# GpSimd's low parts of the second chunk's gate input move ahead of the low parts of a late-weight piece

## The chip, the cores and the metric

The program runs on one core of one Trainium2 chip. The metric is the device time of one execution in microseconds (us), lower is better. A core has a matrix engine (TensorE, PE in the rows), a vector engine (VectorE, DVE), an activation engine (ScalarE, ACT), GpSimd (POOL) and a queue engine (SyncE, SP) that issues transfers between memory and the on-chip SBUF. Each works through its own list of instructions in order, and they wait for one another by semaphores. TensorE writes into PSUM, a second on-chip memory.

## The reference

Three layers follow one another. The first is an attention of 2 × 8 heads over 768 tokens with head size 64, in which a query sees only keys of its own hash bucket. Its output, as 2 × 768 tokens of 512 features, is `x` of the second layer:

```
for k in range(K): gate_pre += conv_w[k] * xp[:, k:k + S, :]   # causal, K = 5 taps
gate = 1.0 / (1.0 + np.exp(-gate_pre))
val = x @ w_val
return gate * val @ w_out
```

The third layer takes that as `x`, with `x_prev` its tokens moved by one:

```
xk = mu_k * x + (1.0 - mu_k) * x_prev
xr = mu_r * x + (1.0 - mu_r) * x_prev
k = np.maximum(xk @ w_k, 0.0)          # 512 -> 1024
v = k * k @ w_v                        # 1024 -> 512
r = 1.0 / (1.0 + np.exp(-(xr @ w_r)))
return r * v
```

## The kernel before

Every fp32 matrix product is made of three products of rounded halves: an operand `a` is split into `a_hi`, a rounded copy, and `a_lo = a - a_hi`, and hi·hi, hi·lo and lo·hi are summed in PSUM. ScalarE makes most high parts, GpSimd most low parts, so each operand of TensorE passes ScalarE and then GpSimd.

The first 245 us or so are the attention, 16 heads in 8 pairs. The rest works on six chunks of 256 tokens, c = 0 to 5. Per chunk TensorE runs, with its matmuls of 128 × 256: **val** (`x @ w_val`, 48 of them), **k** (96), **r** (48), **out** (`y @ w_out`, 48, of the chunk ahead) and **v** (96). Its order is val(0), the last attention product, out(0), then for each c: val(c+1), k(c), r(c), out(c+1), v(c). All three single-pass stages and k share line 702, v is line 710.

Around the change, where attention hands over to the chunks, the work stands so:

- **GpSimd**: the gates of chunks 0 and 1 (`gates`, L416), then the low parts of `y` of chunk 0 (`y_low`, L421, four tiles), with the low parts of pieces 0 and 1 of `w_v` (`w2_low`, L411, one instruction of 128 × 1024 each) put between and behind them, then `x_low(1)` (L358, 128 × 1024), the low part of the second chunk's input, then `s_out(0)` (L432): eight instructions of 128 × 256, `xk_lo` and `xr_lo` by turns for four feature tiles.
- **VectorE**: it normalises the last head (L881), waits for z, and in its own `s_out(0)` runs three instructions for each tile: `tmp_b = z - z_prev` (L958), `tmp_a = mu_k * tmp_b + z_prev` (L960), `tmp_b = mu_r * tmp_b + z_prev` (L963). Later it takes the low parts of pieces 2 and 3 of `w_v` itself (L1006).
- **ScalarE**: `x_hi(1)` (L506), the high part of piece 1 (`w_hi<-w_raw`, L599), then z out of PSUM (L572), `xk_hi` and `xr_hi` (L566), and the high parts of pieces 2 and 3.
- **TensorE**: val(1) waits for `xlo_done`, which `x_low(1)` raises; k(0) waits for `mixlo_done` to stand at 7, so for the last `xk_lo`.
- **SyncE**: `w_v` comes in four pieces of 512 KB through two buffers (L301). Piece n ≥ 2 waits for `w2lo_done[0]` to stand at n - 1: piece 2 for `w2_low(0)`, piece 3 for `w2_low(1)`.

Of the kernel before, what the change touches and what calls it, by code (L numbers as in the profile page):

```python
# [88 lines left out]
def build(nc, qT, kT, v, proj, w1, w2, conv, mu_k, mu_r, codes, rows, out):  # L89
    ctx = ExitStack()  # L90
    with ctx:
# [80 lines left out]
        def w2_piece(halves, n):  # L172
            return halves[n // 2][:, n % 2 * W2_PIECE:(n % 2 + 1) * W2_PIECE]
# [51 lines left out]
        def x_tokens(c, first=HALO):  # L225
            b, n = divmod(c, CPB)
            return x[:, b * DT:(b + 1) * DT, first + n * GQ:first + (n + 1) * GQ]
# [82 lines left out]
        def _(pool):  # L310
# [45 lines left out]
            def x_low(c):  # L356
                pool.wait_ge(xhi_done, c + 1)
                pool.tensor_tensor(x_lo[:, :, :], x_tokens(c), x_hi[:, :, :], ALU.subtract).then_inc(xlo_done, 1)  # L358
# [50 lines left out]
            def w2_low(n):  # L409
                pool.wait_ge(w2hi_done, n + 1)  # L410
                pool.tensor_tensor(w2_piece(w2_lo, n), w2_raw[:, n, :], w2_piece(w2_hi, n), ALU.subtract)\  # L411
                    .then_inc(w2lo_done[0], 1)
# [6 lines left out]
            def y_low(c, m):  # L419
                pool.wait_ge(yhi_done, c * DT + m + 1)  # L420
                pool.tensor_tensor(y_lo[:, m, :], tmp_a[:, m % 2, :], y_hi[:, m, :], ALU.subtract)\  # L421
                    .then_inc(ylo_done, 1)
# [5 lines left out]
            def s_out(c):  # L428
                for m in range(DT):
                    for n, (hi, lo, tmp) in enumerate(((xk_hi, xk_lo, tmp_a), (xr_hi, xr_lo, tmp_b))):  # L430
                        pool.wait_ge(mixhi_done, (c * DT + m) * 2 + n + 1)
                        pool.tensor_tensor(lo[:, m, :], tmp[:, m % 2, :], hi[:, m, :], ALU.subtract)\  # L432
                            .then_inc(mixlo_done, 1)
# [16 lines left out]
            w2_low(0)  # L450
            y_low(0, 2)
            y_low(0, 3)
            w2_low(1)
            pool.wait_ge(mm["val"], DT)
            x_low(1)
            s_out(0)
            for c in range(CHUNKS):
                if c + 1 < CHUNKS:
# [628 lines left out]
```

## Time and profile before

| | |
|---|---|
| time, median of 3 runs | 485.42 us (482.16 to 485.42) |
| the profiled execution's own time | 484.38 us |
| its span in the trace | 482.2 us |
| TensorE busy | 468.8 us, 97% |
| VectorE busy | 352.0 us, 73% |
| ScalarE busy | 274.5 us, 57% |
| GpSimd busy | 252.2 us, 52% |
| chain that ended last | PE 72%, DVE 15%, issue 7%, the rest below 3% each |

The span is from the first to the last instruction in the trace; the execution's own time has 2.2 us more around it. "Busy" counts matmuls that overlap in the pipeline. The granted clock is TensorE's, as a share of full speed (2.4 GHz); 0.50 is its lower level (1.2 GHz). The chain that ended last is followed back from the last instruction, at each step to what released it.

### The profile page before, as it was taken

How to read it: one execution, taken by the hardware profiler on the slowest of the kernel's cores; microseconds unless marked ns; L12 is line 12 of the kernel's file. 1: busy time of each engine (PE TensorE's matmuls, PEld its weight loads, DVE VectorE, ACT ScalarE, POOL GpSimd, SP SyncE). 2: the span in 40 equal slices, each digit the busy share in tenths (PEclk: the TensorE clock that was granted, in tenths of full speed). 3: DMA queues.
4: the chain of work that ended last, by engine and by line, in shares of the span. 5: the costliest groups of instructions: out<-in, count | busy, mean ns of one | idle time of the engine just before them, and what ended most of it. 6: DMA issues, size and time to landing. Idle time of an engine off the chain costs nothing.

```text
span 482.2 us, 9463 instructions
## 1 busy us (share of the span) xinstructions
PE 468.8 (97%) x3493; PEld 398.3 (83%) x3493; DVE 352.0 (73%) x624; ACT 274.5 (57%) x581; POOL 252.2 (52%) x242
## 2 busy tenths in 40 slices
PE   7899999999999999999998999999999999999997
PEld 5766667676676767667778999999999999999997
DVE  5888898989889899888657877876668579326211
ACT  4977877787787887876535541442443353344230
POOL 5786447284553637360377573575455457346140
PEclk9999999999999999999998999999999999999999
DMA  6202414013041311211140001001000000100101
GB/s 231 67 19 71 154 34 153 21 46 131 26 154 35 133 38 29 77 35 34 60 149 2 0 2 45 1 1 44 1 1 27 19 1 2 45 1 1 45 0 46
DMA packets 13885, 23.89 MB, mean 50 GB/s; under 512 B 2960, under 2 KB 10256, under 8 KB 13840
## 3 DMA queue, kind: packets, MB, share of 16 engines
q1 hardware_dynamic: 13552, 23.14, 14.7%
q8 instruction: 28, 0.46, 0.4%
q10 hardware_dynamic: 288, 0.15, 0.1%
q14 instruction: 17, 0.14, 0.1%
HBM read 20.08 MB, written 3.19 MB: 48 GB/s over the span
## 4 chain that ended last, share of the span: by engine, by line
PE 72%; DVE 15%; issue 7%; POOL 2%; ACT 2%; DMA 1%; DVEq 0%; SPq 0%; ACTq 0%; POOLq 0%
PE ps L702 28%; PE ps L710 11%; PE ps L690 11%; PE ps L664 10%; PE ps L675 9%; DVE pt L851 2%; DVE gate L891 2%; DVE negmax L844 2%; DVE k L836 2%; DVE tmp_a L960 2%; DVE tmp_b L958 1%; DVE tmp_b L983 1%; PE ps L647 1%; DVE x L881 1%; PE ps L638 1%
## 5 line engine op out<-in xcount | busy, mean ns | idle before, releaser
L844 DVE TENSOR_REDUCE negmax<-ps 128x1 f32<-128x768 f32 x96 | 91.6, 956 | 16.0 <-PE ps L664 15.3
L484 ACT ACTIVATE probs<-ps,negmax 128x768 f32<-128x768 f32 x96 | 86.6, 902 | 15.7 <-DVE negmax L844 15.4
L664 PE MATMUL ps<-k,q 128*128 128x384 f32 x384 | 92.5, 362 | 3.1 <-ACT probs L484 2.8
L675 PE MATMUL ps<-ident,probs 128*128 128x128 f32 x576 | 83.7, 275 | 2.5 <-DVE pt L851 1.3
L664 PEld LDWEIGHTS ps<-k,q 128*128 128x128 f32 x384 | 62.6, 189 | 24.7 <-ACT probs L484 20.4
L675 PEld LDWEIGHTS ps<-ident,probs 128*128 128x128 f32 x576 | 67.7, 140 | 11.9 <-DVE pt L851 7.5
L690 PE MATMUL ps<-pt,vals 128*64 128x384 f32 x384 | 68.8, 494 | 0.0
L438 POOL TENSOR_TENSOR h_lo<-tmp_b,h_hi 128x256 fp32r<-128x256 f32 x48 | 39.3, 824 | 45.2 <-ACT h_hi L579 45.2
L492 ACT ACTIVATE pt<-ps 128x384 f32<-128x384 f32 x96 | 46.9, 488 | 23.3 <-PE ps L675 21.3
L702 PE MATMUL ps<-xk_hi,w_hi 128*128 128x256 f32 x192 | 54.6, 285 | 1.9 <-POOL xk_lo L432 1.9
L702 PE MATMUL ps<-xk_lo,w_hi 128*128 128x256 f32 x192 | 54.6, 284 | 0.0
L702 PE MATMUL ps<-xk_hi,w_lo 128*128 128x256 f32 x192 | 54.5, 284 | 0.0
L851 DVE COPY pt<-ps 128x384 f32<-128x384 f32 x96 | 52.1, 543 | 2.5 <-PE ps L675 2.5
L710 PE MATMUL ps<-h_hi,w_hi 128*128 128x256 f32 x192 | 53.4, 278 | 0.0
L710 PE MATMUL ps<-h_lo,w_hi 128*128 128x256 f32 x192 | 53.3, 278 | 0.0
L710 PE MATMUL ps<-h_hi,w_lo 128*128 128x256 f32 x192 | 53.3, 278 | 0.0
L891 DVE SCALAR_TENSOR_TENSOR gate<-x,conv_sb,gate 128x256 f32<-128x256 f32 x96 | 50.2, 523 | 1.5
L690 PEld LDWEIGHTS ps<-pt,vals 128*64 128x64 f32 x384 | 24.8, 136 | 31.2 <-issue 31.1
L337 POOL TENSOR_TENSOR q<-raw_q,q 64x768 fp32r<-64x768 f32 x16 | 29.2, 1826 | 39.9 <-DVE gate L891 28.6
L983 DVE TENSOR_TENSOR tmp_b<-tmp_a 128x256 f32<-128x256 f32 x48 | 32.2, 671 | 22.5 <-ACT tmp_a L586 21.8
L702 PEld LDWEIGHTS ps<-xk_hi,w_hi 128*128 128x128 f32 x192 | 37.0, 193 | 2.1 <-POOL xk_lo L432 2.1
L702 PEld LDWEIGHTS ps<-xk_lo,w_hi 128*128 128x128 f32 x192 | 37.2, 194 | 0.0
(84 smaller groups left out, 1090.2 us busy)
## 6 DMA issues: line engine op xcount, KB each, us to landing
w_raw<-w SPq DMA_DIRECT2D x8, 640.0 KB, 5.3
raw_q<-qT SPq DMA_DIRECT2D x8, 384.0 KB, 4.0
raw_k<-kT SPq DMA_DIRECT2D x8, 384.0 KB, 3.7
vals<-v SPq DMA_DIRECT2D x16, 192.0 KB, 2.5
r_sb<-rows SPq DMA_DIRECT2D x32, 96.0 KB, 2.7
out<-w_raw SPq DMA_DIRECT2D x24, 128.0 KB, 1.7
w_raw<-w SPq DMA_DIRECT2D x4, 512.0 KB, 4.2
rows<-r_rows SPq DMA_DIRECT2D x64, 0.8 KB
```

Source lines behind the costliest of these rows:

```text
L438: pool.tensor_tensor(h_lo[:, m, :], tmp_b[:, m % 2, :], h_hi[:, m, :], ALU.subtract)\
L484: act.activation(probs[par][:, :], score[par], ACT.Exp, bias=negmax[:, t:t + 1], accum_out=sums[:, t, 0:1]).then_inc(exp_done, 1)
L492: act.activation(pt[head % 2][:, 0:3, tt * P:(tt + 1) * P], tbank3[0], ACT.Copy).then_inc(up_done[0], 1)
L664: last = pe.matmul(ps[:, 2 * par + half, 0:HALF], qq[h][:, q], kk[h][:, half * HALF:(half + 1) * HALF], start=first, stop=not first)
L675: last = pe.transpose(tbank[u][:, k * P:(k + 1) * P], probs[g % 2][:, kt * P:(kt + 1) * P], ident[:, :])
L690: last = pe.matmul(ps[DH * n:DH * (n + 1), 6, 0:HALF], vals[h][:, kt, :], pt[h][:, kt, n * HALF:(n + 1) * HALF], start=kt == 0, stop=kt == ...
L702: last = pe.matmul(ps[:, bank, 0:GQ], wt[:, w], act_in[:, kt, :], start=(kt == 0 and n == 0), stop=(kt == kts - 1 and n == 2))
L710: last = pe.matmul(ps[:, m, 0:GQ], wt[half][:, first:first + P], act_in[:, kt, :], start=(kt == 0 and n == 0), stop=(kt == FT - 1 and n == 2))
L844: dve.tensor_reduce(negmax[:, t:t + 1], score[g % 2], AX.XY, ALU.max, negate=True).then_inc(max_done, 1)
L851: dve.tensor_copy(pt[head % 2][:, 3:6, tt * P:(tt + 1) * P], tbank3[1]).then_inc(up_done[1], 1)
L891: ins = dve.scalar_tensor_tensor(to, src, conv_sb[:, m, k:k + 1], to, ALU.mult, ALU.add)
L983: dve.tensor_tensor(tmp_b[:, m % 2, :], tmp_a[:, m % 2, :], tmp_a[:, m % 2, :], ALU.mult)\
```

## The change

In GpSimd's list the wait for val(0) and `x_low(1)` stand ahead of `w2_low(1)` and no longer behind it. No instruction is added or removed, and the lists of the other engines are as before.

```diff
@@ -450,9 +450,9 @@
             w2_low(0)
             y_low(0, 2)
             y_low(0, 3)
-            w2_low(1)
             pool.wait_ge(mm["val"], DT)
             x_low(1)
+            w2_low(1)
             s_out(0)
```

GpSimd's list at that place, before; `w_lo<-w_raw,w_hi` is `w2_low`, its first row piece 0 and its second piece 1, `x_lo` is `x_low(1)`:

```order
 L421 TENSOR_TENSOR y_lo<-tmp_a,y_hi 128x256 x2
 L411 TENSOR_TENSOR w_lo<-w_raw,w_hi 128x1024
 L421 TENSOR_TENSOR y_lo<-tmp_a,y_hi 128x256 x2
 L411 TENSOR_TENSOR w_lo<-w_raw,w_hi 128x1024
 L358 TENSOR_TENSOR x_lo<-x,x_hi 128x1024
 L432 TENSOR_TENSOR xk_lo<-tmp_a,xk_hi 128x256
 L432 TENSOR_TENSOR xr_lo<-tmp_b,xr_hi 128x256
```

And the difference that the change makes there, the only one on any engine:

```order
 L411 TENSOR_TENSOR w_lo<-w_raw,w_hi 128x1024
 L421 TENSOR_TENSOR y_lo<-tmp_a,y_hi 128x256 x2
+L358 TENSOR_TENSOR x_lo<-x,x_hi 128x1024
 L411 TENSOR_TENSOR w_lo<-w_raw,w_hi 128x1024
-L358 TENSOR_TENSOR x_lo<-x,x_hi 128x1024
 L432 TENSOR_TENSOR xk_lo<-tmp_a,xk_hi 128x256
 L432 TENSOR_TENSOR xr_lo<-tmp_b,xr_hi 128x256
```

`x_lo` has moved past one instruction and past its wait for piece 1's high part; piece 1's low part now stands behind the wait for val(0) and for `x_hi(1)`.

## Rows read from the trace of the kernel before

**Rows 1.** Waits of TensorE, whole span: who for whom, us in total, times, longest.
```profile
PE ps L664 <- ACT probs L484: 2.8, 3, 1.7
PE ps L702 <- POOL xk_lo L432: 1.9, 1, 1.9
...
PE ps L702 <- ACT recept L595: 0.2, 1, 0.2
```

**Rows 2.** The chain that ended last, 245 to 280: start us, us, what.
```profile
249.25 2.50 DVE tmp_a L960
...
259.35 19.62 PE ps L702 x156
```

**Rows 3.** Timeline of GpSimd: start us, us, what, idle before it and its releaser.
```profile
242.51 1.41 POOL L421 TENSOR_TENSOR y_lo<-tmp_a,y_hi 128x256 fp32r<-128x256 f32 x2
246.52 2.40 POOL L411 TENSOR_TENSOR w_lo<-w_raw,w_hi 128x1024 fp32r<-128x1024 f32 x1 [2.60 <-ACT w_hi L599]
248.88 2.58 POOL L358 TENSOR_TENSOR x_lo<-x,x_hi 128x1024 fp32r<-128x1024 f32 x1
...
258.39 0.91 POOL L432 TENSOR_TENSOR xk_lo<-tmp_a,xk_hi 128x256 fp32r<-128x256 f32 x1
```

**Rows 4.** Timeline of VectorE, chunk 0 and the same step of chunk 1.
```profile
245.38 1.14 DVE L881 TENSOR_TENSOR x<-ps,r_sb 64x384 f32<-64x384 f32 x2 [3.61 <-PE ps L690]
...
247.48 1.73 DVE L958 TENSOR_TENSOR tmp_b<-z 128x256 f32<-128x256 f32 x1 [0.83 <-ACT z L572]
249.25 2.49 DVE L960 SCALAR_TENSOR_TENSOR tmp_a<-tmp_b,mu_sb,z 128x256 f32<-128x256 f32 x1
251.77 0.49 DVE L963 SCALAR_TENSOR_TENSOR tmp_b<-tmp_b,mu_sb,z 128x256 f32<-128x256 f32 x1
...
279.57 2.23 DVE L958 TENSOR_TENSOR tmp_b<-z 128x256 f32<-128x256 f32 x1 [3.43 <-ACT z L572]
281.83 0.48 DVE L960 SCALAR_TENSOR_TENSOR tmp_a<-tmp_b,mu_sb,z 128x256 f32<-128x256 f32 x1
```

**Rows 5.** Timeline of GpSimd in chunk 1's step.
```profile
279.12 2.39 POOL L358 TENSOR_TENSOR x_lo<-x,x_hi 128x1024 fp32r<-128x1024 f32 x1
```

**Rows 6.** Timeline of TensorE at val(1) and k(0).
```profile
250.90 0.28 PE L702 MATMUL ps<-y_hi,w_lo 128*128 128x256 f32 x1
251.51 0.38 PE L702 MATMUL ps<-x_hi,w_hi 128*128 128x256 f32 x1 [0.33 <-POOL x_lo L358]
...
257.15 0.28 PE L702 MATMUL ps<-x_hi,w_lo 128*128 128x256 f32 x1
259.35 0.39 PE L702 MATMUL ps<-xk_hi,w_hi 128*128 128x256 f32 x1 [1.92 <-POOL xk_lo L432]
...
260.28 0.40 PE L702 MATMUL ps<-xk_lo,w_hi 128*128 128x256 f32 x1
...
263.68 0.31 PE L702 MATMUL ps<-xk_hi,w_lo 128*128 128x256 f32 x1
```

**Rows 7.** By stretch: busy us of each engine, then TensorE's granted clock, DMA.
```profile
11.00:13.00 2.00, 0.32 (x3) 0.08 (x1) 2.00 (x3) 1.12 (x3) 2.00 (x2) 1.00 0.00 0
...
260.00:265.00 5.00, 5.00 (x32) 5.00 (x32) 3.21 (x6) 2.51 (x6) 3.19 (x4) 0.66 0.01 3
```

**Rows 8.** Timeline of ScalarE.
```profile
242.13 1.04 ACT L506 ACTIVATE x_hi<-x 128x1024 fp32r<-128x1024 f32 x1
245.39 1.06 ACT L599 ACTIVATE w_hi<-w_raw 128x1024 fp32r<-128x1024 f32 x1 [2.21 <-DMA w_raw<-w]
...
259.07 1.99 ACT L599 ACTIVATE w_hi<-w_raw 128x1024 fp32r<-128x1024 f32 x2
...
277.92 1.05 ACT L506 ACTIVATE x_hi<-x 128x1024 fp32r<-128x1024 f32 x1
```

**Rows 9.** VectorE's normalising line: durations in ns, min/median/max, all 32.
```profile
L881 DVE TENSOR_TENSOR x<-ps,r_sb x32: 549/556/561, 39.9 to 246.0; 64x384 f32<-64x384 f32 x32
```

**Rows 10.** The page's transfer issues: KB each, median us to landing.
```profile
w_raw<-w SPq DMA_DIRECT2D x4, 512.0 KB, 4.2
```

## The prediction

> **What bounds the kernel now.** The table of busy times shows TensorE at 97%, so I first read where it still waits. Its waits over the whole span [rows 1] name, from the hand-over of the attention to the chunks on, only three worth a look: 1.9 us for `xk_lo` at the start of k(0), 0.33 us for `x_lo` at the start of val(1) [rows 6], and 0.2 us for `recept` at out(2). Everything behind k(0) is matmul after matmul, so what k(0) wins in start time comes out at the end, unless a slower loop on the other engines takes it back.
>
> Next, the chain of waits: before k(0) it does not run through TensorE but through VectorE's `tmp_a` (L960) of the first tile, 2.50 us, and after it through 156 matmuls, 19.62 us [rows 2]. The same instruction takes 0.48 us one chunk later [rows 4]. The reader is to see why by laying the timelines of the two engines beside each other [rows 3, 4]. `tmp_b` starts at 247.48, while GpSimd runs `w_lo` (246.52 to 248.92), and ends at 249.21, 0.29 us behind it. `tmp_a` starts at 249.25, while GpSimd runs `x_lo` (248.88 to 251.46), and ends at 251.74, 0.28 us behind it. In chunk 1 there is one long GpSimd instruction only, `x_lo` from 279.12 to 281.51 [rows 5]; there `tmp_b` takes 2.23 us and ends at 281.80, 0.29 us behind it, and `tmp_a` is free. So a VectorE instruction with two SBUF inputs is held until GpSimd's current one is over, and in chunk 0 that happens twice, since two long ones stand back to back. VectorE, ScalarE and GpSimd then run the four tiles to the last `xk_lo`, at 258.39 + 0.91 = 259.30, and k(0) starts at 259.35 [rows 3, 6].
>
> Last, the granted clock by stretches: it is 0.66 of full between 260 and 265 [rows 7], and single matmuls show it: 16 steps from 260.28 to 263.68, 0.2125 us each, against (257.15 - 251.51)/47 = 0.120 in val(1), 0.118 without its first, longer step [rows 6]. That is the lower level, right behind the gap of 1.92 us.
>
> **The change, term by term.** One GpSimd instruction of 2.4 us passes another; nothing is added.
>
> *`x_lo` in its new place.* It needs the y parts before it (over at 243.92, rows 3), `x_hi(1)` (over at 243.17, rows 8) and val(0), which was done before `x_hi(1)` began, since ScalarE waits for it there. GpSimd was idle for 2.60 us just here, waiting for piece 1's high part [rows 3], so `x_lo` runs at 243.9 to 246.3, at 2.39 us [rows 5]; nothing else uses that time. Stretched by 0.2 us, as the 2.58 in its old place, it ends at 246.5.
>
> *`w2_low(1)`.* Its high part is ready at 245.39 + 1.06 = 246.45 [rows 8] and it started at 246.52; between `x_lo`'s end at 246.3 or 246.5 and that there is 0 to 0.2 us left, so it stays where it was, within 0.1. So does the transfer of piece 3 that it releases at 248.92: at 4.2 us to landing [rows 10] it is in by 253.2, while ScalarE takes it up, with all earlier by 2.0, at 257.1 [rows 8]. Cover 3.9 us, cost nothing.
>
> *val(1).* `x_lo` is five us ahead of need. val(1) began 0.61 us behind the last matmul of out(0), where 0.12 is the step: 0.49 earlier. Alone this is worth nothing, because k(0) waits for `xk_lo` and its gap would only grow.
>
> *The first tile on VectorE.* `tmp_b` still sits behind `w_lo` and ends at 249.21; `tmp_a` has no long GpSimd instruction beside it: 0.48 for 2.49, so it ends 2.01 us earlier. Behind it, the cascade keeps its steps if z comes in time: the third z needs the third tile of out(0), whose last matmul is at about 250.90 - 12 × 0.118 = 249.5, and is wanted at 250.6; the fourth has more room. So the last `xk_lo` ends at 257.3 and k(0) starts at 257.35: **-2.0 us**. The bounds: nothing, if the hold isn't what makes `tmp_a` long, and -2.0; I take the latter, as chunk 1 shows this very pair of instructions with one hold.
>
> *The gap and the clock.* TensorE's last val(1) matmul starts at 256.66, 0.49 earlier, and ends at 256.94. The gap is 0.4 us instead of 1.92. I expect no fall of the clock behind it: 16 matmuls win 0.0945 each, -1.5. Against that stands the spacing of the matmuls that follow: 132 steps from 263.68 to the last of the 156 took 0.1137 each [rows 2, 6], closer than the 0.118 of val(1), and I can't tell whether that comes back without the fall. At 0.118 throughout, the 156 take 156 × 0.118 + 0.3 = 18.7 for 19.62: **-0.9 us**; at 0.1137 it is 18.0: -1.6. I take the first, from the stretch nearest in kind and time. If the clock falls all the same, the term is 0.
>
> *The loop behind it.* VectorE's square steps of k(0) and its low parts move by 2.0 with the start, the rest by what TensorE gives: it was idle 3.43 us before the first z of out(1) [rows 4], and 2.4 of it stay, so z sets its pace there, and that follows TensorE through ScalarE's `x_hi(2)` (1.05 us, rows 8). Both then are 2.9 to 3.0 earlier, and the 0.2 us at out(2) stays what it was, give or take. Behind that nothing is changed.
>
> Sum: -2.0 - 0.9 = **-2.9 us**, so 481.5 for the profiled execution (span 482.2 to 479.3, own time 484.38). The median of the runs is 1.04 above that execution: 485.42 - 2.9 = **482.5 us**.
>
> **Rivals.**
>
> 1. *The clock falls all the same*, somewhere in k(0). For: one fall after one gap is a thin base, and in the first 15 us a gap of 1.7 us (the longest for `probs`, rows 1) left the clock at 1.00 [rows 7], so the gap of 1.92 alone may not be the cause. Against: no fall is to be seen in any stretch where TensorE is not held. Only the -2.0 is left: 483.4. The Trainium skill (TensorE: Matmul & The Clock Gate, "Why this matters for your kernels") warns only of idle gaps clearly longer than the one here, so by it this gap didn't bring the clock down and closing it needn't keep it up; no run yet shows which.
>
> 2. *The fall is worth more.* The runs lie 3.3 us apart. If the lowest is one without a fall in k(0), and after the change all are like it, they come to 482.16 less the 2.0 of the hold: 480.2, with the closer spacing 480.0. For: a spread of this size fits one or two falls of 1.5. Against: nothing in one profile says which runs had them.
>
> 3. *The hold isn't the cause, or moves on*: `tmp_a` stays at 2.5. Then val(1) is early, k(0) starts as before, gap 2.4: 485.4. Against it stand three instructions that end 0.28 to 0.29 us behind GpSimd's.
>
> 4. *Slower: the normalising step is held instead.* VectorE's L881 starts its two halves at 245.38, now beside `x_lo`. If its first half waits for `x_lo` and its second for `w_lo`, it ends at 248.92 + 0.56 = 249.5. TensorE wants it for the third tile of out(0) at 250.90 - 23 × 0.118 = 248.2. From there on it decides: idle 1.3 us, and if the clock falls for that gap too, 1.5 more; val(1)'s last matmul is at 256.66 + 2.8 = 259.5, k(0) starts at 259.6 for 259.35, and with the fall in k(0) as before the end is 485.7. Against: its 32 instructions take 549 to 561 ns, held by none of GpSimd's [rows 9]; one of their two inputs is in PSUM. The Trainium skill (GPSIMD Engine Reference, "Key points") names contention for VectorE instructions with two SBUF inputs, and that would leave this one alone; the rows agree.
>
> **Chances and range.** Forecast 0.57; rival 1, 0.18; rival 2, 0.15; rival 3, 0.07; rival 4, 0.03. The change lies between 0 and -5.2 us. A measurement of this kernel tells about 1% (4.9 us) from no change. Only rival 2 gets past it, and not always, since its 480.0 to 480.2 is just past 480.6: faster 0.13. Slower by 1% has no case: 0.02. Same 0.85. The range takes in the forecast with both spacings (481.8 to 482.5), rival 1 and rival 2, and stops short of rival 3, but with the runs' own scatter: 480.0 to 484.8.
>
> **What would show it.** `x_lo` at 243.9 and `w_lo` still at 246.5 on GpSimd; `tmp_a` at 0.5 us; k(0) from 257.3 behind a gap of 0.4; clock 1.00 between 258 and 263; out(1)'s first z about 3 us earlier; the wait at out(2) still small. Wrong would be: `tmp_a` still 2.5 us (rival 3), 16 matmuls at 0.21 (rival 1), normalising above 0.56 us (rival 4), or a wait at out(2) of over 0.5, where the loop of the other engines keeps what TensorE won.

## The result, and the profile after

The changed kernel takes 481.14 us (median of 20 runs, 480.35 to 484.0), the kernel before in the same measurement 484.22 us (20 runs, 482.16 to 486.7). The ratio is 0.9942, 95% interval 0.9929 to 0.9955, so 2.8 us less, 2.2 to 3.4; forecast was 2.9 less, 482.5 in a range of 480.0 to 484.8. Two later measurements of the same kernel gave 0.9945 (0.9929 to 0.9961) and 0.9966 (0.9946 to 0.9986), so 2.7 and 1.6 us less; the interval of the last ends at 2.6. The forecast time is 1.4 above the measured one, because it was built on the three runs before, whose median of 485.42 lies 1.2 above that of the twenty. The profiled execution has a span of 479.2 us for 482.2 and a time of 481.46 for 484.38.

TensorE's waits in the changed kernel (who for whom, us in total, times, longest) answer to [rows 1]:

```profile
PE ps L664 <- ACT probs L484: 2.8, 3, 1.7
...
PE ps L702 <- POOL xk_lo L432: 0.6, 1, 0.6
...
PE ps L702 <- ACT recept L595: 0.2, 1, 0.2
```

The wait for `xk_lo` is down from 1.9 to 0.6, that for `x_lo` is gone. The timeline of GpSimd, as [rows 3]:

```profile
243.09 1.41 POOL L421 TENSOR_TENSOR y_lo<-tmp_a,y_hi 128x256 fp32r<-128x256 f32 x2
244.46 2.39 POOL L358 TENSOR_TENSOR x_lo<-x,x_hi 128x1024 fp32r<-128x1024 f32 x1
246.80 2.41 POOL L411 TENSOR_TENSOR w_lo<-w_raw,w_hi 128x1024 fp32r<-128x1024 f32 x1
250.54 0.92 POOL L432 TENSOR_TENSOR xk_lo<-tmp_a,xk_hi 128x256 fp32r<-128x256 f32 x1 [1.33 <-ACT xk_hi L566]
```

`x_lo` fills most of the 2.60 us in which GpSimd had waited for piece 1's high part (from 244.46, not 243.9, as the `y` parts end later here), and `w_lo` follows 0.28 us later than before. The timeline of VectorE, as [rows 4]:

```profile
245.58 1.15 DVE L881 TENSOR_TENSOR x<-ps,r_sb 64x384 f32<-64x384 f32 x2 [3.61 <-PE ps L690]
...
247.68 1.81 DVE L958 TENSOR_TENSOR tmp_b<-z 128x256 f32<-128x256 f32 x1 [0.82 <-ACT z L572]
249.52 0.48 DVE L960 SCALAR_TENSOR_TENSOR tmp_a<-tmp_b,mu_sb,z 128x256 f32<-128x256 f32 x1
```

`tmp_b` still ends 0.28 us behind `w_lo`; `tmp_a` takes 0.48 for 2.49. The normalising step ran beside `x_lo` at its usual length. TensorE at k(0) and out(1), as [rows 6], and the busy time by stretches, as [rows 7]:

```profile
257.64 0.38 PE L702 MATMUL ps<-xk_hi,w_hi 128*128 128x256 f32 x1 [0.61 <-POOL xk_lo L432]
...
273.97 0.28 PE L702 MATMUL ps<-xr_hi,w_lo 128*128 128x256 f32 x1
274.42 0.36 PE L702 MATMUL ps<-y_hi,w_hi 128*128 128x256 f32 x1 [0.17 <-ACT recept L595]
```

```profile
257.00:260.00 3.00, 2.39 (x21) 2.36 (x21) 1.34 (x4) 2.93 (x5) 1.55 (x3) 1.00 0.00 0
260.00:265.00 5.00, 5.00 (x46) 5.00 (x45) 4.15 (x5) 1.50 (x4) 3.58 (x4) 1.00 0.02 3
```

Between 260 and 265 the granted clock is 1.00 for 0.66, and 46 matmuls run for 32. Last, ScalarE from the end of k(0)'s h steps to the first z of out(1). The h steps square k(0)'s result on VectorE and split it on ScalarE and GpSimd; `recept` is r's result on its way out of PSUM:

```profile
273.58 0.42 ACT L579 ACTIVATE h_hi<-tmp_b 128x256 fp32r<-128x256 f32 x1 [0.32 <-DVE tmp_b L983]
273.91 1.19 ACT L595 ACTIVATE recept<-ps 128x256 f32<-128x256 f32 x4
274.96 1.09 ACT L506 ACTIVATE x_hi<-x 128x1024 fp32r<-128x1024 f32 x1
276.13 0.39 ACT L572 ACTIVATE z<-ps 128x256 f32<-128x256 f32 x1
```

Nothing here waits for TensorE any longer: the four `recept` follow the last h step, and `x_hi` and z follow them.

### The profile page after: what moved, and what is told of

The parts are those of the page before. It is cut to its first block, busy times and chain, and to the rows that moved or that the text cites. A ratio compares the mean times of both kernels' runs of the same rounds, so it can differ in the third digit from the quotient of the medians.

```text
span 479.2 us, 9463 instructions
## 1 busy us (share of the span) xinstructions
PE 467.7 (98%) x3493; PEld 397.1 (83%) x3493; DVE 349.9 (73%) x624; ACT 274.2 (57%) x581; POOL 251.7 (53%) x242
## 4 chain that ended last, share of the span: by engine, by line
PE 69%; DVE 17%; issue 7%; POOL 2%; ACT 2%; DMA 2%; DVEq 0%; SPq 0%; ACTq 0%; POOLq 0%
PE ps L702 24%; PE ps L710 11%; PE ps L690 11%; PE ps L664 10%; PE ps L675 9%; DVE gate L891 2%; DVE pt L851 2%; DVE tmp_b L983 2%; DVE negmax L844 2%; DVE tmp_b L958 2%; DVE k L836 2%; DVE tmp_a L960 1%; PE ps L647 1%; DVE x L881 1%; PE ps L638 1%
```

## The experiments

The eleven kernels are compared by the starts in one profile for each measurement (us; "out(0) to k(0)" and "loop" are spans from start to start). "Loop" is from the first z of out(1) to the first `recept` of chunk 1, "rest" from out(2) to the end. TensorE's waits at k(0) are the "gap". The last column counts the runs whose mean granted clock was 0.996 or less (one of change_beside has 0.993), the others having 0.999 or 1.000; in the profiles that have 0.996 (before, hold_back) that is one fall of 3.4 us, at k(0). In the other runs the place of a fall, and the length of the gap, are not on record.

| kernel | out(0) | k(0) | out(0) to k(0) | gap | z of out(1) | loop | out(2) | rest | runs with a fall |
|---|---|---|---|---|---|---|---|---|---|
| before | 245.26 | 259.35 | 14.09 | 1.92 | 279.06 | 37.57 | 317.14 | 165.0 | 14 of 31, 9 of 20, 8 of 18, 5 of 11 |
| changed | 245.46 | 257.64 | 12.18 | 0.61 | 276.13 | 37.54 | 314.18 | 165.0 | 3 of 20 |
| hold_back | 245.61 | 259.39 | 13.78 | 2.21 | 279.03 | 37.54 | 317.08 | 165.3 | 9 of 12 |
| hold_half | 245.12 | 258.16 | 13.04 | 1.47 | 276.55 | 37.52 | 314.58 | 165.3 | 0 of 11 |
| gap_filled_before | 245.27 | 259.00 | 13.73 | 0.45 | 277.53 | 37.55 | 315.60 | 165.0 | 0 of 12 |
| behind_both | 245.03 | 256.44 | 11.41 | none | 275.09 | 37.60 | 313.20 | 165.0 | 1 of 9 |
| change_again | 245.53 | 257.66 | 12.13 | 0.56 | 276.19 | 37.52 | 314.22 | 165.0 | 0 of 6 |
| gap_filled_after | 245.16 | 257.16 | 12.00 | none | 275.79 | 38.73 | 315.03 | 164.8 | 1 of 12 |
| low3_late | 245.32 | 257.12 | 11.80 | 0.22 | 275.19 | 38.27 | 313.97 | 164.8 | 1 of 9 |
| change_beside | 245.36 | 257.29 | 11.93 | 0.36 | 275.63 | 38.48 | 314.62 | 164.8 | 2 of 12 |
| nudged | 245.78 | 257.79 | 12.01 | 0.44 | 276.28 | 37.55 | 314.34 | 165.5 | 0 of 6 |
| behind_both_again | 245.26 | 256.67 | 11.41 | none | 275.46 | 38.45 | 314.42 | 165.0 | 0 of 7 |
| four_out | 245.19 | 256.99 | 11.80 | 0.22 | 275.32 | 37.56 | 313.39 | 164.8 | 0 of 5 |
| four_out_behind | 245.16 | 256.57 | 11.41 | none | 275.22 | 37.54 | 313.27 | 165.0 | 0 of 6 |

**hold_back: the second hold put back.** Piece 1's low part is taken twice.

```diff
             def w2_low(n):
                 pool.wait_ge(w2hi_done, n + 1)
+                if n == 1:
+                    part = W2_PIECE
+                    pool.tensor_tensor(w2_lo[0][:, W2_PIECE:W2_PIECE + part], w2_raw[:, 1, 0:part],
+                                       w2_hi[0][:, W2_PIECE:W2_PIECE + part], ALU.subtract).then_inc(again, 1)
+                    pool.wait_ge(again, 1)
```

> The changed kernel, with piece 1's low part taken twice on GpSimd, so that a second instruction of 2.4 us again stands behind the first while VectorE has its first tile in hand; x_lo and val(1) stay early. Theory (the two-input VectorE instruction is held by GpSimd's current one, and the second hold was the 2.0 us): tmp_a is 2.4 to 2.5 us again, the gap before k(0) grows to 2.6 to 2.8 us, the clock falls behind it, time as before the change, 484 to 485 (ratio to before 0.999 to 1.002). Rival (the gain came from val(1)'s early start, or from anything else in x_lo's new place): 481 to 482, ratio 0.994.

Measured: 484.28 us, ratio 1.0013 (0.9996 to 1.0029); the gap is 2.21 us, a little less than foretold. Its timelines of GpSimd and VectorE:

```profile
246.58 2.39 POOL L414 TENSOR_TENSOR w_lo<-w_raw,w_hi 128x1024 fp32r<-128x1024 f32 x1
249.04 2.46 POOL L417 TENSOR_TENSOR w_lo<-w_raw,w_hi 128x1024 fp32r<-128x1024 f32 x1
```

```profile
247.83 1.42 DVE L964 TENSOR_TENSOR tmp_b<-z 128x256 f32<-128x256 f32 x1 [0.83 <-ACT z L578]
249.28 2.50 DVE L966 SCALAR_TENSOR_TENSOR tmp_a<-tmp_b,mu_sb,z 128x256 f32<-128x256 f32 x1
```

In the measured time the whole gain is gone, though `x_lo` and val(1) stayed early. From out(0) to k(0) 1.60 of the 1.91 us are back; the other 0.3 is missing because the second long instruction ends 0.3 earlier against out(0) than in the kernel before (251.50 - 245.61 for 251.46 - 245.26). The hold is the cause, and val(1)'s early start is worth nothing by itself.

**hold_half: half of it.** The same edit with `part = W2_PIECE // 2`.

> The same with a second instruction of half the width, about 1.2 us. Theory of the hold: tmp_a about 1.3 to 1.4 us, k(0) starts 0.9 to 1.2 later than in the changed kernel, gap 1.5 to 1.8; time 482.1 if the clock stays up through that gap, 483.3 if it falls (ratio to before 0.996 or 0.998). Rival: 481 to 482 as for the full one, tmp_a 0.5.

Measured: 482.18 us, ratio 0.9963 (0.9948 to 0.9979), and no fall in any of 11 runs. The instruction times were foretold wrong: the half stands first, so it holds `tmp_b`, and the whole one behind it holds `tmp_a`:

```profile
247.34 0.68 DVE L964 TENSOR_TENSOR tmp_b<-z 128x256 f32<-128x256 f32 x1 [0.83 <-ACT z L578]
248.05 2.50 DVE L966 SCALAR_TENSOR_TENSOR tmp_a<-tmp_b,mu_sb,z 128x256 f32<-128x256 f32 x1
```

The two together come to 3.2 us, against 2.3 in the changed kernel and 3.9 in hold_back, and k(0) moves by as much. What counts is when the last long GpSimd instruction is over: k(0) starts 7.89 us behind its end in the kernel before, in hold_back and in hold_half (258.16 for 250.27).

**gap_filled_before: the clock alone.** The kernel before, with TensorE's gap filled; the results are overwritten.

```diff
             def s_k(c):
 
+                if c == 0:
+                    pe.wait_ge(z_done, 1)
+                    for n in range(15):
+                        pe.matmul(ps[:, 4, 0:GQ], w1_hi[:, n * P:(n + 1) * P], x_hi[:, n % DT, :], start=True, stop=True)
```

> The kernel before with 15 matmuls put into TensorE's gap between val(1) and k(0), their results overwritten; the two holds stay. It prices the clock alone. Theory: k(0) starts at 259.4 as before, the clock stays at 1.00, and 0.9 us (spacing 0.118) to 1.6 us (0.1135) are won: 482.6 to 483.3, ratio 0.9965 to 0.998. If the fall costs nothing at the end, or the loop of the other engines keeps it: ratio 1.000.

Measured: 482.62 us, ratio 0.9976 (0.9963 to 0.9988). None of 12 runs has a fall, where 14 of 31 of the kernel before beside it have one. In those 31 the ones with a fall have a median of 484.30, the others of 482.96: a fall costs 1.3 us, and it is a draw of each execution. k(0) itself did not start at 259.4 as foretold but at 259.00, since piece 1's high part was there earlier in this execution and `w_lo` began at 246.14; so the two profiles differ by more than the clock, and the price of the fall is taken from the medians. Its profile, where the kernel before had 0.66:

```profile
260.00:265.00 5.00, 5.00 (x46) 5.00 (x45) 3.22 (x6) 2.15 (x5) 3.55 (x4) 1.00 0.02 3
```

**behind_both: no long instruction beside the first tile.**

```diff
+        def w2_from(n):
+            return w_raw[:, 0:W2_PIECE] if n == 3 else w2_raw[:, n % 2, :]
...
-                if n >= 2:
-                    sp.wait_ge(w2lo_done[0], n - 1)
+                if n == 2:
+                    sp.wait_ge(w2lo_done[0], 1)
+                if n == 3:
+                    sp.wait_ge(wlo_done, 2 * PAIRS)
+                    sp.wait_ge(w2_in[1], 16)
...
             x_low(1)
-            w2_low(1)
             s_out(0)
+            w2_low(1)
```

> A further step: piece 3 of the late weights is loaded into another free buffer (so it no longer waits for piece 1's low part), and piece 1's low part is taken by GpSimd behind the eight xk_lo/xr_lo. No long GpSimd instruction then stands beside the first tile. Theory: tmp_b 0.42 too, the last xk_lo 1.4 earlier, TensorE has no gap at k(0) and wins the 0.6 that is left; but GpSimd's low part pushes y_lo of chunk 1 back by 0.7 to 1, and the h loop with it, so that out(1) waits: 480.5 to 481.5, ratio to before 0.992 to 0.9945. Rival (the loop is not near the end of its slack): 480.3, ratio 0.992.

Measured: 480.68 us, ratio 0.9941 (0.9921 to 0.9961). Both holds are off:

```profile
247.25 0.42 DVE L964 TENSOR_TENSOR tmp_b<-z 128x256 f32<-128x256 f32 x1 [0.83 <-ACT z L578]
247.71 0.48 DVE L966 SCALAR_TENSOR_TENSOR tmp_a<-tmp_b,mu_sb,z 128x256 f32<-128x256 f32 x1
```

k(0) now follows val(1) without a gap. That is the end of what this place can give: 0.8 us of k(0)'s start against the change. Two thirds of it are lost again in k(0) and r(0), whose matmuls here follow one another at the wider of two spacings (more on them under nudged):

```profile
256.44 0.28 PE L708 MATMUL ps<-xk_hi,w_hi 128*128 128x256 f32 x1
...
273.28 0.28 PE L708 MATMUL ps<-xr_hi,w_lo 128*128 128x256 f32 x1
```

These are 16.84 us for the 143 steps that take 16.33 in the changed kernel (257.64 to 273.97). All profiles divide this way at k(0): behind a gap of 0.22 to 1.47 us the spacing was 0.1133 to 0.1135 us (eight profiles), and so it was behind the fall in the other two that have a gap; without a gap it was 0.1177 (four: behind_both twice, four_out_behind, gap_filled_after). Closing the gap entirely so costs 0.5 us there. In other stages a gap doesn't decide it, out(1) behind one ran at either spacing, and no run shows why.

**change_again and gap_filled_after: the falls that are left.** The second is the changed kernel with the edit of gap_filled_before, 5 matmuls for 15.

> The changed kernel once more, as the measure for the three beside it. Ratio to before 0.993 to 0.9955. How often its runs show a mean granted clock of 0.996 (a fall of the clock in them) is the question: 3 of 20 so far. If the gap of 0.6 us at k(0) is what brings those falls, about the same again.

> The changed kernel with 5 matmuls in the gap of 0.6 us that is left before k(0). Theory (the falls that are left in some runs come from that gap): none of its runs has a fall, median as the undisturbed runs of the change, 481.0, ratio 0.993 to 0.995. Rival (they come from elsewhere in the kernel): 1 or 2 runs in 10 still show 0.996 and lie 2.5 us above the others.

Measured: 481.43 us, ratio 0.9945 (0.9929 to 0.9961), and 481.92 us, ratio 0.9963 (0.9951 to 0.9975). One of 12 runs without a gap still has a fall, so the few that the changed kernel has need not come from its gap; the rival stands but for the price (that run lies 1.5 us above the others), and no profile caught one. Why the filled kernel is the slower one, its profile suggests twice: k(0) and r(0) took the wider spacing, and its loop took 38.73 us for 37.54, with 1.11 us of waiting for an output transfer in it, of which more below.

**low3_late: does the loop keep part of the gain?**

```diff
                 if c == 0:
-                    w2_low()
+                    w2_low(2)
                 s_k(c)
+                if c == 0:
+                    w2_low(3)
```

> The changed kernel, with VectorE's low part of piece 3 (1.7 us) taken behind the square steps of k(0) and no longer ahead of them. It asks what the loop of the other engines kept. Theory (the h steps end last at out(1), where TensorE waits 0.17 us): that wait goes, recept is there 1.5 us earlier, and 0.2 us are won at most, since TensorE is next; but the moved piece now lies against GpSimd's recept and x_lo, which end 0.3 to 0.7 later and with them the held tmp_b, so that out(2) waits longer: in all 480.8 to 481.6, within 0.1% of the change. Rival (the loop set the pace all along): 480.0 or less.

Measured: 481.59 us, ratio 0.9956 (0.994 to 0.9973). The wait at out(1) is gone and z comes at 275.19, 0.94 earlier, but out(2) only 0.21. Beside the moved piece GpSimd's `recept` step took 1.59 us for 1.05, so `x_lo` starts only 0.40 earlier, at 275.80 for 276.20. `tmp_b` now begins ahead of it, and `tmp_a` is held where `tmp_b` was. The two end 0.2 us later behind z for that, and 0.41 of the 0.73 us by which the loop is longer is a wait for an output transfer:

```profile
275.70 0.43 DVE L958 TENSOR_TENSOR tmp_b<-z 128x256 f32<-128x256 f32 x1 [0.79 <-ACT z L572]
276.17 2.51 DVE L960 SCALAR_TENSOR_TENSOR tmp_a<-tmp_b,mu_sb,z 128x256 f32<-128x256 f32 x1
```

**nudged: the spacing of matmuls.** One matmul of 64 columns ahead of k and r from chunk 1 on, and of val from chunk 2 on:

```diff
+            def nudge(bank, act_in):
+                pe.matmul(ps[:, bank, 0:64], w1_hi[:, 0:P], act_in[:, 0, 0:64], start=True, stop=True)
```

> The changed kernel with one extra matmul of 64 columns ahead of val, k and r of each chunk from 1 on (its result is overwritten). Matmuls follow one another at 0.1134 or at 0.1178 us, stage by stage, and nothing in the rows says why. If a short disturbance at a stage's start sets the closer spacing, up to 192 x 5 x 0.0044 = 4 us are won: 477 to 479. If not: 481 plus 14 x 0.03 to 0.06, 481.5 to 481.9.

Measured: 482.07 us, ratio 0.9963 (0.9949 to 0.9977), 0.6 above change_again on the same chip: about the price foretold for the extra matmuls, though the intervals of the two overlap. Single stages did change (val(2), val(3), two k stages and r(5) to the closer spacing, v(5) to the wider), most not. What sets the spacing is open.

**change_beside and behind_both_again: on one chip.**

> The changed kernel, as the measure for the one beside it on the same chip: ratio to before 0.993 to 0.9955.

> The kernel with piece 1's low part behind the eight xk_lo/xr_lo once more, to be compared with the change on one chip. Its k(0) starts 1 us earlier in the trace than the change's, its out(2), from which the rest takes 165 us in every trace so far, 1.0 earlier. Theory (out(2)'s start, set by the loop of the other engines, sets the end): 0.5 to 1.0 us below the change in the median. Rival: no difference, 0.2 or less.

Measured: 481.93 us, ratio 0.9966 (0.9946 to 0.9986), and 481.52 us, ratio 0.9948 (0.9929 to 0.9966). The difference of 0.4 is below what the intervals resolve. But the profiles show what blurs it. VectorE's third output product of chunk 0 in change_beside, and in behind_both_again:

```profile
292.35 0.42 DVE L1000 TENSOR_TENSOR w_raw<-ps,recept 128x256 f32<-128x256 f32 x1 [0.81 <-DMA out<-w_raw]
```

```profile
292.12 0.42 DVE L1006 TENSOR_TENSOR w_raw<-ps,recept 128x256 f32<-128x256 f32 x1 [0.74 <-DMA out<-w_raw]
```

It waits for the first product's transfer, since there are two output buffers, and the loop grew from 37.5 to 38.5 us. That the chunks run earlier doesn't explain it: without the wait the third product follows the first by 3.27 us in every profile, before (291.59, 294.87) as after (288.66, 291.93), and behind_both, with the earliest z of all at 275.09, has no wait. What differs is the first transfer, issued between 287.5 and 289.3. Its KB and us from issue to landing, in the first profile of the change and in change_beside:

```profile
out<-w_raw SPq DMA_DIRECT2D x1, 128.0 KB, 1.8
```

```profile
out<-w_raw SPq DMA_DIRECT2D x1, 128.0 KB, 3.6
```

It took 3.6 us in behind_both_again, 3.9 in gap_filled_after and 3.2 in low3_late, and the waits of 0.81, 0.74, 1.11 and 0.41 us go with it; in behind_both it took 1.7. Queue, packets, MB and share of the 16 engines from 289.4 to 290.6, in the same two profiles:

```profile
q1 hardware_dynamic: 144, 0.13, 32.4%
q8 instruction: 1, 0.02, 6.8%
```

```profile
q1 hardware_dynamic: 135, 0.12, 29.8%
q8 instruction: 1, 0.02, 7.0%
```

A 16 KB packet of the instruction queue passes among the packets of the first product's transfer. In the four profiles with the wait (change_beside, behind_both_again, gap_filled_after, low3_late) it starts 0.22 to 0.31 us behind the first of them, and the last nine of the 144 start 0.7 to 1.3 us after the others, in change_beside at 291.09 for 289.97. In the two profiles of the change without the wait it starts 0.58 to 0.59 us behind, when all 144 have started. No experiment moved that packet, so this cause is read from the traces and not shown by a run.

**four_out and four_out_behind: that wait taken away.** Applied to the change and to behind_both.

```diff
-        o_out = w_raw[:, 0:2 * GQ].rearrange("p (s q) -> p s q", q=GQ)
+        o_out = w_raw[:, 0:4 * GQ].rearrange("p (s q) -> p s q", q=GQ)
...
-                    wait(dve, out_done[m % 2], (c * DT // 2 + m // 2) * 16)
+                    wait(dve, out_done[m], c * 16)
```

> The changed kernel with four output buffers in place of two. In some executions of the change VectorE's third product of chunk 0 waited 0.8 us for the first product's output transfer, and out(2) came 0.9 later against out(1)'s z. Theory (that wait is what the loop keeps of the gain in those): no such wait, z of out(1) to the first recept of chunk 1 is 37.5 to 37.6 in every profile, out(2) at 313.9 to 314.2, median 480.6 to 481.2, ratio 0.993 to 0.9945, the runs closer together. Rival (something else stretches the loop): unchanged, 481.1 to 481.9 with z to recept of 38.5 possible.

> Four output buffers, and piece 1's low part behind the eight xk_lo/xr_lo. Theory: the 0.7 to 1.0 us that this order wins at z of out(1) now stays to the end in every run: out(2) at about 313.2, 480.2 to 480.6, ratio to before 0.991 to 0.9935. Rival: as the kernel beside it, within 0.2 us.

Measured: 480.52 us (480.45 to 481.04, 5 runs), ratio 0.9942 (0.9928 to 0.9956), and 480.55 us (480.49 to 480.72, 6 runs), ratio 0.994 (0.9927 to 0.9954). No VectorE wait for an output transfer is left in either profile around chunk 0's products, the loop is 37.56 and 37.54 us, and the runs lie within 0.6 us, where the three measurements of the change had even their fall-free runs 1.3 to 1.8 us apart. Both have the lowest medians of all, four_out's below the 480.6 to 481.2 foretold, but by the ratios neither is shown faster than the change. In four_out the first transfer was slow too, 4.0 us with nine late packets, and no product waited for it. behind_both's order adds nothing to four buffers: 0.03 us between the medians where 0.7 to 1.0 were foretold, so the rival holds. In their profiles z was only 0.10 us apart, as four_out's k(0) was early itself and at the closer spacing.

## Why the prediction was right, by its own steps

*`x_lo` in its new place*: right; 2.39 us in GpSimd's idle time, though 0.5 us later than forecast. *`w2_low(1)`* stayed, 0.28 us later and not within 0.1, of which 0.2 is the whole trace's (out(0) starts at 245.46 for 245.26). *val(1)* early is worth nothing alone: hold_back.

*The first tile, -2.0*: right. From out(0) to k(0) it is 12.18 us for 14.09, 1.91 less, and putting the hold back takes 1.60 of it away. Where both kernels' clocks are on record in one measurement, the runs without a fall have medians of 483.40 before and 481.44 after, and of 483.34 and 481.78: 2.0 and 1.6 us.

*The gap and the clock, -0.9*: the sum came out, the term was put together wrongly. In the traces' own time k(0) is 1.71 us earlier (0.2 of the 1.91 are given up ahead of out(0)) and z of out(1) 2.93, so this term measured 1.2; it and the first are each off by 0.3, and the errors cancel. Three things were wrong in it. First, it took the fall for a fixed part of the kernel before. It is a draw: 36 of 80 runs, 0.9 to 1.3 us each between the medians of the four comparisons, and the profiled execution happened to be one. In the medians the falls are thus worth about 0.4 to 0.5 us and not 0.9 (483.82 for all runs before against 483.40 without a fall, and 483.82 against 483.34), so that 2.8 us came out in the first measurement, with 2.7 and 1.6 in the others, is in part luck. The change makes the fall rare, 3 of 20, 0 of 6 and 2 of 12; the first rival was right that it can happen all the same, but not as the usual case. Second, the closer spacing did come back, as at every k(0) behind a gap: from 257.64 to 273.97 are 143 steps, 0.1142 each, where I had taken 0.118. TensorE could have begun out(1) at 274.08, one step behind 273.97, 3.4 us earlier than before, where I had 2.9. Third, it could not use that: it waited 0.17 us for `recept` and began at 274.42.

*The loop*: here the step failed in its reason. I wrote that z follows TensorE and 2.4 us of VectorE's idle time stay. 2.21 stay, and z is set by ScalarE, whose `recept` runs right behind the h steps. Those had moved by 1.7 us only (273.91 for 275.61, the first `recept` in each). z moved by 2.93 because the wait for TensorE that stood between them is gone, 0.98 us at the fourth `recept`, and a little idle time with it. In the kernel before:

```profile
275.61 1.05 ACT L595 ACTIVATE recept<-ps 128x256 f32<-128x256 f32 x3
277.64 0.38 ACT L595 ACTIVATE recept<-ps 128x256 f32<-128x256 f32 x1 [0.98 <-PE ps L702]
```

So TensorE's gain and the loop's lay within 0.5 us of each other, and the lesser one came through. Loop and rest are then as before, 37.54 and 165.0 us, which is why 2.9 at z became 3.0 at the end. That out(2) plus 165 us is the end, in all profiles within 164.8 to 165.5, shows where any further gain has to arrive.

*Rivals*: the second, all runs without a fall at 480.2, took the lowest run as its base, where the fall-free ones before have medians of 482.96 to 483.40; the change's are at 481.03 to 481.78. The third is refuted by `tmp_a` at 0.48 and by hold_back, the fourth by the normalising step, 1.15 us beside `x_lo`. As for the gap and the clock, of the two kernels whose profile has a gap of 1.9 to 2.2 us 45 of 92 runs have a fall (36 of 80, 9 of 12), filling the gap left none in 12, and the kernel with 1.47 us has none in 11. The page of the Trainium skill that I had set against it (TensorE: Matmul & The Clock Gate, "Why this matters for your kernels") warns of longer gaps only; here the shorter ones already do it in half of the runs, and the measurement decides.

## What to carry to other kernels

Lay the timelines of VectorE and GpSimd beside each other: where a VectorE instruction with two SBUF inputs ends a fixed 0.28 us behind a long GpSimd one, it was held, and two long ones back to back hold two. The short ones hold as well, but only for their own length. Put long GpSimd work where VectorE works out of PSUM or idles, ahead of the short steps on the path rather than beside them. Whether a fall of the clock in one profile belongs to every execution or is a draw, only the mean clock of many runs tells; and after a gain, look for the loop with the least slack, since what TensorE wins beyond it isn't paid out.

## What the runs showed of the hardware

- A two-input VectorE instruction waits for GpSimd's current one and gets in before the next: `tmp_b` 0.42 us with nothing beside it (behind_both), up to 2.23 us behind `x_lo`; `tmp_a` 0.48 to 2.51. GpSimd's next one, already begun, then takes longer: 2.58 us for 2.39 (`x_lo` in the kernel before). Instructions of 0.92 us hold too: in the second tile before, `tmp_a` takes 0.84 us and ends at 253.47, 0.28 behind `xk_lo`. With an input in PSUM it isn't held (1.14 and 1.15 us for the normalising pair, alone and beside `x_lo`).
- TensorE's clock fell to its lower level at gaps of 1.9 to 2.2 us in about half of the executions, not in all; in hold_back's profile it fell at 259.38, with the gap's end at 259.39, in the kernel before at 260.28, 0.9 us behind it. Kernels whose profiles have no such gap show falls too, 8 in 115 runs, 2.6 us dear in the change (483.67 against 481.03) and 1.5 in gap_filled_after; where they lie is open.
- Matmuls of 128 x 256 follow one another at 0.1134 or 0.1178 us for a whole stage, 4% apart, at the same granted clock. At k(0) it was the closer one behind a gap in all ten profiles that have a gap, and the wider one in all four that have none.
- The output transfer of 128 KB takes 1.7 to 2.1 us in the median of chunk 0's four, but the first of them took 3.2 to 4.0 in five profiles, in which nine of its packets started 0.7 to 1.3 us behind the rest, with a 16 KB packet of the instruction queue beside them. With two output buffers VectorE waited 0.41 to 1.11 us for it, with four it didn't wait. That this packet is the cause is argued only.
